# The first supertile of a fused attention and two-layer MLP kernel in another order: attention over four bank pairs, weight sums on VectorE, high parts 6 blocks ahead

## What is computed

```python
# q, k, v: batch 8, heads 8, sequence 576, head dimension 64; chunks of 64
scores = scale * np.matmul(q_c, k_c.transpose(0, 1, 2, 4, 3))
scores = scores - np.max(scores, axis=-1, keepdims=True)
attn = np.exp(scores); attn = attn / (np.sum(attn, axis=-1, keepdims=True) + 1e-09)
x = concat_heads(np.matmul(attn, v_c))            # 4608 tokens x 512
h = x @ w_in                                      # 512 -> 2048
x = (np.maximum(h, 0.0) + alpha * np.minimum(h, 0.0)) @ w_out      # 2048 -> 512
h = x @ w2_in
out = (h - np.tanh(h)) @ w2_out
```

## Time and profile before

| | us |
|---|---|
| median of 3 runs | 1648.54 |
| the runs | 1644.33, 1648.54, 1649.12 |
| the profiled execution | 1645.04 |
| its span | 1643.2 |
| TensorE busy | 1584.7 (96%) |
| VectorE, ScalarE, GpSimd busy | 977.2, 671.3, 328.6 |

### The profile page before, as it was taken

One profiled execution on the slowest core, in us unless ns is written; L12 is line 12 of the kernel. 1 busy time (PEld: TensorE's weight loads), 2 busy tenths in 40 slices (PEclk: granted clock), 3 DMA queues, 4 the chain that ended last, 5 costly groups with the idle time before them and its releaser, 6 DMA issues.

```text
span 1643.2 us, 26691 instructions
## 1 busy us (share of the span) xinstructions
PE 1584.7 (96%) x10512; PEld 1487.1 (90%) x10512; DVE 977.2 (59%) x1351; ACT 671.3 (41%) x995; POOL 328.6 (20%) x454
## 2 busy tenths in 40 slices
PE   4879999999999999999999999999999999999999
PEld 3878899989999999999989988988988988988987
DVE  5557868766785776676674562562662562562542
ACT  4566535535553554554553241242232232232221
POOL 3684556676564200000000000000000000000000
PEclk9999999999999999999999999999999999999999
DMA  5477688769879756755734843853853843843842
GB/s 206 170 280 251 232 311 339 263 238 363 277 251 333 285 181 215 269 175 183 298 140 152 311 178 129 330 181 127 334 180 124 334 178 125 335 175 127 295 178 76
DMA packets 72938, 375.04 MB, mean 228 GB/s; under 512 B 9072, under 2 KB 13168, under 8 KB 38256
## 3 DMA queue, kind: packets, MB, share of 16 engines
q1 hardware_dynamic: 63216, 341.87, 57.7%
q0 software_dynamic: 9600, 31.46, 5.2%
HBM read 308.29 MB, written 65.01 MB: 227 GB/s over the span
## 4 chain that ended last, share of the span: by engine, by line
PE 86%; DVE 4%; DMA 3%; POOL 3%; issue 2%; ACT 2%; SPq 0%; ACTq 0%; POOLq 0%; DVEq 0%
PE banks L522 13%; PE banks L523 13%; PE banks L524 13%; PE banks L551 7%; PE banks L553 7%; PE banks L552 7%; PE banks L585 5%; PE banks L586 5%; PE banks L584 5%; PE a_bank L584 3%; PE a_bank L585 3%; PE a_bank L586 3%; DMA raw<-in_weights 2%; POOL ring L339 1%; DVE go_lo L960 1%
## 5 line engine op out<-in xcount | busy, mean ns | idle before, releaser
L522 PE MATMUL banks<-xo_hi,ring 128*128 128x384 f32 x1344 | 453.4, 337 | 20.1 <-POOL ring L339 7.6
L524 PE MATMUL banks<-xo_hi,ring 128*128 128x384 f32 x1344 | 452.2, 336 | 0.0
L523 PE MATMUL banks<-xo_lo,ring 128*128 128x384 f32 x1344 | 452.1, 336 | 0.0
L960 DVE TENSOR_TENSOR go_lo<-g_full,go_hi 128x768 fp32r<-128x768 f32 x288 | 287.1, 999 | 252.1 <-ACT go_hi L746 251.4
L746 ACT CAST go_hi<-g_full 128x768 fp32r<-128x768 f32 x288 | 239.6, 837 | 366.3 <-PE banks L586 223.5
L551 PE MATMUL banks<-go_hi,ring 128*128 128x384 f32 x768 | 265.6, 346 | 13.9 <-DVE go_lo L960 8.7
L522 PEld LDWEIGHTS banks<-xo_hi,ring 128*128 128x128 f32 x1344 | 254.6, 189 | 24.7 <-POOL ring L339 14.4
L553 PE MATMUL banks<-go_hi,ring 128*128 128x384 f32 x768 | 257.0, 335 | 0.0
L552 PE MATMUL banks<-go_lo,ring 128*128 128x384 f32 x768 | 256.8, 334 | 0.0
L523 PEld LDWEIGHTS banks<-xo_lo,ring 128*128 128x128 f32 x1344 | 254.6, 189 | 0.4
L524 PEld LDWEIGHTS banks<-xo_hi,ring 128*128 128x128 f32 x1344 | 254.5, 189 | 0.0
(11 more groups left out here) (98 smaller groups left out, 1924.1 us busy)
## 6 DMA issues: line engine op xcount, KB each, us to landing
ring<-w_split SPq DMA_DIRECT2D x242, 1024.0 KB, 5.5
qkv<-in_chunks SPq DMA_DIRECT2D x60, 384.0 KB, 5.0
w_split<-ring SPq DMA_DIRECT2D x22, 1024.0 KB, 5.1
w_split<-made_first POOLq DMA_DIRECT2D x44, 256.0 KB, 5.8
w_split<-sums POOLq DMA_DIRECT2D x44, 256.0 KB, 5.6
y_between<-stage SPq DMA_DIRECT2D x12, 768.0 KB, 7.2
x_raw<-y_between SPq DMA_DIRECT2D x6, 1536.0 KB, 9.4
out<-x_raw SPq DMA_DIRECT2D x36, 256.0 KB, 6.6
```

Source lines behind the costliest of these rows:

```text
L522: nc.tensor.matmul(h, hi, xo_hi[:, o, k, :], start=fresh and k == 0, stop=False, skip_group_check=not fresh)
L523: nc.tensor.matmul(h, hi, xo_lo[:, o, k, :], start=False, stop=False, skip_group_check=not fresh)
L524: last = nc.tensor.matmul(h, lo, xo_hi[:, o, k, :], start=False, stop=k == 1, skip_group_check=not fresh)
L960: nc.vector.tensor_tensor(go_lo[:, slot, :, :], g_of(n), go_hi[:, slot, :, :], ALU.subtract).then_inc(glo_ready, 1)
```

## The change

It touches the opening and run 0 alone.

- **Attention of the opening.** `probs` gets two more places in `stage` (`probs_first`), so units 0 to 3 each have their own; units 4 and 5 take the places of units 0 and 1, and wait for those units' transposes. Units 4 and 5 take the bank pairs of units 0 and 2. The order of scores, transposes and outputs, of exponents, copies and high parts, and of shifts and normalizations is written out anew.
- **Weight sums.** GpSimd makes those of pairs 0 and 1. Those of pairs 2 to 7 are made by VectorE, between c12(p-1) and u3(p) for pair p+2. S2 and S3 of odd pairs go to `made_first`, so that two pairs' sums can be there at once.
- **High parts.** In phase A of run 0, ScalarE goes to base(p)+5 before the copy s1(p), to base(p)+9 after reading c11(p-1), and to base(p)+11 after reading the rest of pair p-1. The opening leaves block 9 as the last, where it was 13. Phase B still goes 10 blocks ahead.

```diff
-AHEAD = 10
+AHEAD, NEAR = 10, 6
...
         attnT_first = stage[:, 0:2 * G * UNIT * P].rearrange("x (s b n) -> x s b n", s=2, b=G * UNIT)
+        probs_first = stage[:, 2 * G * UNIT * P:4 * G * UNIT * P].rearrange("x (s b r j) -> x s b r j", s=2, b=G * UNIT, r=2)
...
-                return banks[:, 2 * (u % 4) - 2:2 * (u % 4), :] if u % 4 else a_bank
+                pair = u if u < 4 else (0, 2)[u - 4]
+                return banks[:, 2 * pair - 2:2 * pair, :] if pair else a_bank
...
+        def probs_of(u):
+
+            return probs_first[:, u % 4 - 2, :, :, :] if opening(u) and u % 4 >= 2 else probs[:, u % 2, :, :, :]
+
+        def probs_users(u):
+
+            return u - 3 if opening(u) else u - 1
+
+        def sum_of(name, p):
+
+            if name == "S4":
+                return sums[:, 2 + p % 2, :]
+            i = {"S2": 0, "S3": 1}[name]
+            return more_sums[:, i, :] if p % 2 else sums[:, i, :]
...
+            weight_sums(0)
             for j in range(BLOCKS):
-                what, i, p = block_use(0, j)
-                if what == "product" and i == (6 if p else 1):
-                    weight_sums(0, j, p)
+                if j == product_at(0, 2, 0):
+                    weight_sums(1)
...
-                        pe.wait_ge(x_copied, u - 3)
+                        pe.wait_ge(x_copied, (1, 3)[u - 4])
...
-            for u in range(4):
-                scores(u)
+            scores(0)
+            scores(1)
+            scores(2)
             transpose_attn(0)
-            for u in range(UPS):
-                if 1 <= u <= 2:
-                    scores(u + 3)
-                output(u)
-                if u + 1 < UPS:
-                    transpose_attn(u + 1)
+            scores(3)
+            output(0)
+            transpose_attn(1)
+            output(1)
+            transpose_attn(2)
+            scores(4)
+            output(2)
+            transpose_attn(3)
+            scores(5)
+            output(3)
+            transpose_attn(4)
+            output(4)
+            transpose_attn(5)
+            output(5)
...
-                high_parts(s, AHEAD)
+                high_parts(s, NEAR)
...
-                    high_parts(s, base(p) + 1 + AHEAD)
+                    high_parts(s, base(p) - 1 + NEAR)
...
-                    high_parts(s, base(p) + 3 + AHEAD)
+                    high_parts(s, base(p) + 3 + NEAR)
                     act_rest(s, p - 1)
-                    high_parts(s, base(p) + 6 + AHEAD)
+                    high_parts(s, base(p) + 5 + NEAR)
                 act_c11(s, PAIRS - 1)
...
             exponent(0)
+            exponent(1)
+            place_attnT(0)
+            exponent(2)
+            copy_x(0)
             high_parts(0, 1)
-            for u in range(UPS):
-                if u + 1 < UPS:
-                    exponent(u + 1)
-                place_attnT(u)
-                copy_x(u)
-                high_parts(0, 3 + 2 * u)
-                if u == 3:
-                    high_x(0, B11)
-                    high_x(0, B21)
+            place_attnT(1)
+            high_parts(0, 3)
+            copy_x(1)
+            exponent(3)
+            place_attnT(2)
+            exponent(4)
+            copy_x(2)
+            high_parts(0, 4)
+            high_x(0, B11)
+            high_x(0, B21)
+            place_attnT(3)
+            exponent(5)
+            copy_x(3)
+            high_parts(0, 7)
+            place_attnT(4)
+            copy_x(4)
+            high_parts(0, 9)
+            place_attnT(5)
+            copy_x(5)
...
+                if probs_users(u) > 0:
+                    dve.wait_ge(attnT_done, probs_users(u))
...
+            def weight_sums(p):
...
+                s2, s3, s4 = sum_of("S2", p), sum_of("S3", p), sum_of("S4", p)
+                dve.wait_ge(raw_in[p % 2], 32 * raw_loads(0, p))
+                if p >= 2:
+                    dve.wait_ge(wlo_ready, product_at(0, 7, p - 2) + 1)
+                nc.vector.tensor_tensor(s3, a11, a21, ALU.subtract).then_inc(w_sum, 1)
+                dve.wait_ge(w_sum, 4 * p + 1)
+                nc.vector.tensor_tensor(a21, a21, a22, ALU.add).then_inc(w_sum, 1)
+                dve.wait_ge(w_sum, 4 * p + 2)
+                nc.vector.tensor_tensor(s2, a21, a11, ALU.subtract).then_inc(w_sum, 1)
+                dve.wait_ge(w_sum, 4 * p + 3)
+                if p >= 2:
+                    dve.wait_ge(wlo_ready, product_at(0, 3, p - 2) + 1)
+                nc.vector.tensor_tensor(s4, a12, s2, ALU.subtract).then_inc(w_sum, 1)
...
+                    if s == 0 and p + 2 < PAIRS:
+                        weight_sums(p + 2)
                     sum_u3(s, p)
                     sum_c22(s, p)
...
             shift(0)
-            for u in range(UPS):
-                if u + 1 < UPS:
-                    shift(u + 1)
-                normalize(u)
+            shift(1)
+            normalize(0)
+            shift(2)
+            normalize(1)
+            normalize(2)
+            shift(3)
+            shift(4)
+            normalize(3)
+            normalize(4)
+            shift(5)
             low_x(0, B11)
+            normalize(5)
             low_x(0, B21)
```

## The result

| | before | after |
|---|---|---|
| median | 1646.72 | 1656.75 |
| lowest, highest (6 runs each) | 1644.31, 1649.12 | 1655.64, 1659.85 |
| the profiled execution, its span | 1645.04, 1643.2 | 1659.85, 1658.1 |
| TensorE busy | 1584.7 | 1592.4 |

The change made the kernel slower by 10.0 us, a ratio of 1.0065 with a 95% interval of 1.0049 to 1.0082. The prediction was 1652.3, +5.5 us, in a range of 1644 to 1660. The direction is right, the size about half of what came. The profiled execution of after is the longest of its runs; the two profiled executions differ by 14.8 us, of which 10.0 are there by unit 4's product (145.25 against 135.25), the place where the prediction made its sum.

What follows compares the result with a forecast made beforehand. The prediction took phase A's ring of waits, not TensorE, to bound phase A, and TensorE the kernel from 500 us on; opening -8.4, ring and clock +11.6, phase B +2.3 gave +5.5 on 1646.8: 1652.3 us, range 1644 to 1660.

Steps and rivals of the forecast that it cites:

- The opening: Attention of the first supertile: last copy of x ends 5.3 us earlier, at 35.9; block 4 starts 8.4 earlier, at 44.6.
- Rival (d): Opening: no gain, as other waits take over; only T1's 3 us remain; 1657.6; chance 0.10 together with rival (c).
- The ring: Phase A of run 0: each load waits through VectorE's sums and activation and ScalarE's c11 read; 12.2 us a pair.
- rival (b): Phase A: same long ring with quick landings, 3.6 us; 11.5 a pair, +2.7, 1649.5; chance 0.27 with what lies near.
- rival (c): Phase A: hindrance of sums by low parts, and clock; +1.3 us a pair, 1657.4; chance 0.10 together with Rival (d).
- The clock: Phase A: TensorE at the 1.2 GHz level after idle time, hidden inside the ring, costs 1.7 us once after the last sums.
- The step into phase B: Start of phase B: at unit 0 ScalarE must take high parts 59 to 65, before 64 and 65 only; +2.3 us.
- The sum: Whole kernel: unit 4's product at 140.8 against 135.25, +5.5 us, so 1652.3; chance of the long ring as forecast 0.50.
- rival (a): Phase A: short ring, c11's wait not coming last; 8.3 us a pair, -10.1, 1636.7; chance 0.13.

Runs made afterwards that it cites:

- run 0: Not a follow-up run but a stretch of the kernel itself, following the opening, with a phase A and a phase B; it has no measured time of its own.
- run 9: The changed kernel with VectorE's four sums moved behind the activation of its pair, high parts still 6 ahead: 1639.95 us, ratio 0.9964.
- run 2: The changed kernel with phase A's high parts 10 ahead again, new opening and sums on VectorE kept: 1634.32 us, ratio 0.9911.
- run 12: The changed kernel with high parts 10 ahead and VectorE's sums behind the activation: 1636.03 us, ratio 0.9941.
- run 5: The kernel before with only phase A's high parts 6 ahead, its own opening and sums on GpSimd: 1652.13 us, ratio 1.0033.
- runs 6 and 7: The changed kernel with high parts in phase B min(10, 4 + n), then min(10, 4 + n // 3) blocks ahead: 1657.60 and 1661.32 us.
- run 1: The changed kernel with ScalarE's high parts up to base(p)+9 ahead of its read of c11: 1650.17 us, ratio 1.0011.
- run 8: The kernel of run 2 with the stores of six groups issued behind the next load of raw slices: 1637.52 us, ratio 0.9947.

## Why the prediction was half right

**The opening** was placed 5.3 us earlier for the last copy of x (35.9 at its end) and 8.4 at block 4. Measured: it starts at 34.09 and ends at 34.68, and block 4 is at 43.31, 9.7 ahead. The stepping by rows of before held to 1.3 us. (Two of its sums are slightly off and decide nothing: the terms given as 8.7 us add up to 8.5, and the three waits given as 7.5 us to 7.2.) T1's high part had nothing ahead of it, as foreseen. Rival (d) is out.

**The ring** was put at 12.2 us a pair. Measured are 12.64 (first sums 54.64 to 105.20, four pairs), with the links in the predicted order. From issue to the first sum I had 4.3; the five measured are 3.46, 4.71, 5.45, 4.06 and 3.38, 4.2 in the mean. The rest was put at 7.9 and is 8.3, 8.0, 8.0 and 8.8. So rival (b), landings of 3.6, is out.

The last first sum is at 105.20 where 105.4 was forecast, and that is partly luck: the first one came 2.0 us early (54.64 for 56.6), and the four pairs took 1.8 us more than 4 x 12.2. Block 42 then starts 3.76 us behind it instead of 2.35, at 108.96 for 107.75. This is of rival (c): in two of the five turns two or three of VectorE's four sums met low parts and took twice as long. In the last turn the four took 3.15 us instead of 1.80. VectorE's timeline of after has one of them:

```profile
106.66 0.83 DVE L951 TENSOR_TENSOR made_first<-raw 128x256 f32<-128x256 f32 x1
```

**The clock** was to cost 1.7 us once after the last sums. It cost 1.6: from 108.96 on matmuls start 0.32 apart for 3.5 us and then 0.17 apart, and block 52, ten blocks later, is at 121.04, which is 1.6 more than ten times 1.045. I had 120.0. So at the end of phase A the forecast is off by 1.0 us. By its terms: opening -9.7 for -8.4, ring and clock +14.0 for +11.6.

**The step into phase B is the term that was mis-sized**: +2.3 predicted, +5.7 measured. The mechanism was right: seven high parts in a row between the two parts of g, with three landings. ScalarE's timeline has them:

```profile
126.85 0.41 ACT L687 CAST ring<-raw 128x256 fp32r<-128x256 f32 x1 [1.94 <-DMA raw<-in_weights]
...
127.91 0.83 ACT L770 CAST go_hi<-g_full 128x768 fp32r<-128x768 f32 x1
128.64 0.41 ACT L687 CAST ring<-raw 128x256 fp32r<-128x256 f32 x1
130.41 0.71 ACT L687 CAST ring<-raw 128x256 fp32r<-128x256 f32 x2 [1.36 <-DMA raw<-in_weights]
133.20 0.71 ACT L687 CAST ring<-raw 128x256 fp32r<-128x256 f32 x2 [2.08 <-DMA raw<-in_weights]
136.62 0.71 ACT L687 CAST ring<-raw 128x256 fp32r<-128x256 f32 x2 [2.70 <-DMA raw<-in_weights]
137.23 0.83 ACT L770 CAST go_hi<-g_full 128x768 fp32r<-128x768 f32 x1
```

The landing that I had at 124.9 is used at 126.85. The last of the seven high parts ends at 137.3 instead of 133.1, and from the end of the part of g (138.1) to unit 4's product it takes 7.2 us instead of 6.8.

The landings are less than half of this. The four loads were issued at 123.93, 126.73, 130.36 and 132.36, and used after 2.92, 3.68, 2.84 and 4.26 us: 3.4 in the mean, where I had 3.3. The two that the chain of waits goes through make 1.3 us more than two of 3.3. The other part is GpSimd's low parts, which must be done before a load may go:

```profile
121.49 5.22 POOL ring L354 x5
126.73 0.33 SPq L1165
127.10 3.21 DMA raw<-in_weights
...
130.89 1.45 POOL ring L354 x2
132.36 0.33 SPq L1165
132.73 3.79 DMA raw<-in_weights
```

In the ring four low parts took 2.8 us, so five would take 3.5; here they took 5.2, while VectorE made low parts of g and an activation beside them (from 120.95, 122.28 and 124.96 on). The low part of block 54 was done at 123.9, where I had 121.5; 1.0 of that was inherited. So the hindrance between the two engines, which I counted in rival (c) for phase A alone, was put at nothing in this term. The traces show it; no run takes it away by itself.

**The sum** is then 1.0 us from block 52, 3.4 from the step: +10.0 at unit 4 in place of +5.5, and +10.0 in the medians. Beyond unit 4 the delay stayed, as forecast. The further 4.8 us between the two profiled executions are not in the medians. In the traces they lie before 586 us: in the 40 us from 185.25 on the mean granted clock is 0.96, where the same stretch of before has 1.00, and from 265 to 585 us TensorE is idle 2.7 us more than before in the stretch 10 us earlier. I have no cause for them.

**The rival (a)** had about the right number for what the change could have been, but not by its terms, since no ring that was cut reached its 8.3 us a pair in the mean: run 9, whose ring is that of (a), is at 1639.95, and run 2 at 1634.32, on either side of the 1636.7 worked out. What decided between it and the forecast was the order of two queues, and it could be read in the code before anything ran.

## What to carry to other kernels

When work is handed to an idle engine, look at what stands behind it in that engine's queue, and follow each waiter until the chain comes to an end or comes back: here it came back to its own load, and sums taken off the ring's GpSimd link, with a shorter distance, made a pair of 10.1 us one of 12.6. Then cut such a ring in one place; a second cut can make a new wait (run 12). Where a distance of preparation is shortened, count what must be caught up later: here it cost 5.4 us by itself (run 5), and putting it elsewhere gave nothing back (runs 6 and 7).

## What the runs showed of the hardware

**Two engines on one memory.** A sum of 128x256 takes VectorE 0.42 us (23 of the 24 sums in run 2 took 0.42 or 0.43), and up to 0.83 to 0.96 where GpSimd's low parts run beside it; GpSimd's low part then takes 0.90 to 0.97, alone 0.73. Both engines lose in such a stretch, but not by every instruction. These rows are of after, VectorE's and GpSimd's timeline of the same moment; the first low part keeps its 0.74 beside a sum that takes 0.96:

```profile
105.66 0.96 DVE L949 TENSOR_TENSOR raw<-raw 128x256 f32<-128x256 f32 x1
```

```profile
105.60 0.74 POOL L354 TENSOR_TENSOR ring<-raw,ring 128x256 fp32r<-128x256 f32 x1 [3.81 <-ACT ring L687]
106.30 0.91 POOL L354 TENSOR_TENSOR ring<-sums,ring 128x256 fp32r<-128x256 f32 x1
```

The Trainium skill ("GPSIMD Engine Reference", its table of the engine) says that VectorE instructions with two SBUF inputs contend for GpSimd's shared interfaces; the traces agree (0.96 for 0.42 on VectorE, 0.91 for 0.73 on GpSimd). The same holds for VectorE's activation: its two halves take 1.94 us in before, and 2.43 in run 9 at 72.24, where a low part beside them took 1.27.

**Landings.** The same load, two slices for one pair, took between 3.2 (run 1) and 7.5 us (run 8) from issue to first sum for pairs 3 to 7 in the kernels with sums on VectorE. What else was queued is the likely reason, but not a shown one: a few of these times hold a wait for VectorE itself, and run 8, which moved the stores, didn't shorten them together. A mean of 4.2 to 4.3 was good enough for the pairs of phase A.

**The clock.** After each of the five idle times of 2.4 to 4.3 us in phase A, TensorE's matmuls started 0.32 us apart for 3 to 6 us, with the granted clock at 0.50, the 1.2 GHz level. In three of the five it stood there from the first matmul after the wait; after the waits of 3.42 and 3.59 us it fell 0.6 and 1.6 us later. Inside the ring this cost nothing, since TensorE was early anyway; after the last turn it cost 1.6 us.
